# A gated-memory mixer and two MLPs on one core: the decay-and-rotation chain in fourteen steps instead of sixteen, with the pair of chunks ahead of the last one

## The reference

```python
def _attn_ref(q, k, v, a_re, a_im):                 # B, H, S, D = 4, 8, 768, 48
    mag = np.sqrt(a_re * a_re + a_im * a_im)
    scale = np.minimum(mag, 0.999) / (mag + 1e-06)
    a_re_n, a_im_n = (a_re * scale, a_im * scale)
    for t in range(S):
        ar, ai = (a_re_n[:, :, t, :, None], a_im_n[:, :, t, :, None])
        new_re = ar * S_re - ai * S_im
        new_im = ar * S_im + ai * S_re
        kv = np.einsum('bhd,bhe->bhde', k[:, :, t], v[:, :, t])
        S_re, S_im = (new_re + kv, new_im)
        y[:, :, t] = np.einsum('bhd,bhde->bhe', q[:, :, t], S_re)
def _moe_ref(x, w_in, w_out):                       # 3072 tokens, 384 -> 2048 -> 384
    h = x @ w_in
    g = h * np.clip(h + 3.0, 0.0, 6.0) / 6.0
    return g @ w_out
def _moe2_ref(x, w1, w2, w3, w_out):                # 384 -> 1024 twice, product, 1024 -> 1024 -> 384
    h = ((x @ w1) * (x @ w2)) @ w3
    return h @ w_out
```

## Time and profile before

| what | us |
|---|---|
| median of 3 runs (lowest, highest) | 1022.08 (1019.12, 1023.35) |
| the profiled execution's own time | 1022.37 |
| its span, first to last instruction | 1020.6 |
| busy: TensorE, VectorE, ScalarE, GpSimd | 910.4, 470.5, 430.5, 256.6 |
| first matmul of the first MLP | 101.53 |
| first MLP, units 0 to 7 | 101.53 to 712 |
| second MLP | 712 to 1020.6 |

### The profile page before, as it was taken

One profiled execution on the slowest core, in us unless ns is written; L12 is line 12 of the kernel. 1 busy time (PEld: TensorE's weight loads), 2 busy tenths in 40 slices (PEclk: granted clock), 3 DMA queues, 4 the chain that ended last, 5 costly groups with the idle time before them and its releaser, 6 DMA issues.

```text
span 1020.6 us, 14665 instructions
## 1 busy us (share of the span) xinstructions
PE 910.4 (89%) x5721; PEld 834.9 (82%) x5721; DVE 470.5 (46%) x610; ACT 430.5 (42%) x650; POOL 256.6 (25%) x200
## 2 busy tenths in 40 slices
PE   6944469889989989989989989989999999999996
PEld 3534468879889889889889889989888888888886
DVE  6445549849658648648748733233212121212110
ACT  4543535555655655555555532353212122212121
POOL 1011336222222222222222222343222222222221
PEclk9977769989989999999999999999999999999999
DMA  9584132353343343343344141510101010101000
GB/s 347 201 230 128 46 63 78 85 119 88 108 87 95 100 91 98 93 90 99 107 89 110 48 84 50 188 68 11 44 1 62 1 62 1 62 1 62 1 32 33
DMA packets 73688, 85.85 MB, mean 84 GB/s; under 512 B 6928, under 2 KB 59792, under 8 KB 73616
## 3 DMA queue, kind: packets, MB, share of 16 engines
q1 hardware_dynamic: 73216, 84.07, 29.7%
q10 hardware_dynamic: 400, 0.80, 0.5%
...
## 4 chain that ended last, share of the span: by engine, by line
issue 39%; PE 38%; POOL 14%; DVE 3%; ACT 2%; DMA 2%; SPq 1%; ACTq 0%; POOLq 0%; DVEq 0%
POOL gL L1328 13%; PE hb L937 10%; PE acc L959 7%; PE bQ L937 5%; PE bR L937 5%; PE bP L959 2%; PE hb L796 2%; PE acc L816 2%; PE acc L890 2%; DMA F<-QKs 1%; PE hb L890 1%; DVE QKc L1198 1%; DMA wo_sb<-in_moe_w_out_dram 1%; PE bQ L846 0%; PE bR L846 0%
## 5 line engine op out<-in xcount | busy, mean ns | idle before, releaser
L1328 POOL TENSOR_TENSOR gL<-g_sb,gH 128x384 fp32r<-128x384 f32 x128 | 157.1, 1227 | 428.2 <-ACT gH L1036 425.9
L796 PE MATMUL hb<-xHL,winH 128*128 128x384 f32 x768 | 168.6, 356 | 10.7 <-DMA xHL<-yHL 9.1
L816 PE MATMUL acc<-gH,woutH 128*128 128x384 f32 x384 | 134.0, 349 | 32.5 <-POOL gL L1328 23.6
L1237 DVE SCALAR_TENSOR_TENSOR g_sb<-t_sb,hb 128x384 f32<-128x384 f32 x128 | 70.4, 550 | 189.6 <-ACT t_sb L1046 105.8
L796 PEld LDWEIGHTS hb<-xHL,winH 128*128 128x128 f32 x768 | 140.2, 199 | 13.3 <-DMA xHL<-yHL 9.5
L1046 ACT ACTIVATE t_sb<-hb,cst 128x384 f32<-128x384 f32 x128 | 74.4, 581 | 154.1 <-PE hb L796 153.4
L816 PE MATMUL acc<-gH,woutL 128*128 128x384 f32 x384 | 133.3, 347 | 0.0
L816 PE MATMUL acc<-gL,woutH 128*128 128x384 f32 x384 | 132.8, 346 | 0.0
L1341 POOL TENSOR_TENSOR pL<-p_sb,pH 128x512 fp32r<-128x512 f32 x48 | 67.0, 1396 | 231.9 <-ACT pH L1098 231.9
L816 PEld LDWEIGHTS acc<-gH,woutH 128*128 128x128 f32 x384 | 75.0, 195 | 37.6 <-issue 29.3
L1036 ACT CAST gH<-g_sb 128x384 fp32r<-128x384 f32 x128 | 65.3, 510 | 79.4 <-DVE g_sb L1237 79.2
...
## 6 DMA issues: line engine op xcount, KB each, us to landing
...
```

Source lines behind the costliest of these rows:

```text
L796: mm = pe.matmul(o, w[:, kk * DF1 + ft * P:kk * DF1 + (ft + 1) * P], xv(u)[:, 2 * kk + part, :], start=(i == 0), stop=(i == 8))
L816: mm = pe.matmul(acc[m][:, 0:UNIT], w[:, ft * DM + m * P:ft * DM + (m + 1) * P], gg[:, (n % 3) * UNIT:(n % 3 + 1) * UNIT], start=(ft == 0 ...
L1237: dve.scalar_tensor_tensor(out=g_sb[:, :], in0=t_sb[:, :], scalar=6.0, in1=hb[n % 2][:, 0:UNIT], op0=ALU.min, op1=ALU.mult).then_inc(s["hs ...
L1328: pool.tensor_tensor(gL[:, (n % 3) * UNIT:(n % 3 + 1) * UNIT], g_sb[:, :], gH[:, (n % 3) * UNIT:(n % 3 + 1) * UNIT].bitcast(F32), ALU.subt ...
```

## The change

- The chain takes steps 0 to 13. ScalarE and VectorE's steps are dealt out anew: the arctangent moves from step 10 to 6, the sum of the angles from 11 to 7, the wrapped turns from 12 to 8 and 9, the exponentials of the magnitudes stand at 9, cos at 10, sin at 11.
- A fourth work tile, `W4`, holds the angles. For units 0 and 1 it lies over `gH` (`W4_early`), which the first MLP does not use yet; from unit 2 on it is `x2_sb`, the tile in which the first MLP's output is copied out. So there are new waits: the first three `gH` wait for unit 1's wrapped turns, `evac_x2_act` waits for the wrapped turns of a unit, and step 3 waits until `x2_sb` has been stored.
- The factor 1/pi was a ScalarE pass (L1020); it is now inside VectorE's instructions, which are one pass more.
- "Pairs first": the products with decays, cos and sin are done for chunks 0 and 1 at steps 10 and 12 and for chunk 2 at steps 11 and 13. The loads of q and k are split likewise: one DMA for the pair, one for the last chunk, in place of one for q and one for k.
- In a slot ScalarE does relu, `gH`, chunk work, chain step; VectorE does `g_sb`, chunk work, chain step.
- SyncE issues both halves of the pair scatter at step 13 and loads the next AR, AI at step 11; the store of the first MLP's output stands at slot 2, not 3.
- Units 0 and 1 of the chain, the splits of weights and the rows of `w3 @ w_out` stand at other slots; in unit 7 the second MLP's weights are split in halves over six slots.

```diff
+        W4_early = at("W4_early", KT * UNIT, F32, where[0] - 4 * (KT * UNIT + 6 * UNIT))
...
-        SPLIT_H = {(-1, 0): (0,), (-1, 8): (4,), (-1, 9): (1,), (0, 1): (5,), (0, 3): (2,), (0, 5): (6,), (0, 7): (3,), (0, 9): (7,)}
+        SPLIT_W = {(-2, 15): (0,), (-1, 3): (1,), (-1, 8): (4,), (0, 0): (2,), (0, 2): (5,), (0, 4): (3,), (0, 6): (6,), (0, 8): (7,)}
...
             if u == -1:
-                return ([(1, 0)] if sl == 0 else []) + ([(1, sl + 1)] if sl < 9 else [])
+                return [(1, sl)] if sl <= 10 else []
             if u == 0:
-                return {0: [(1, 10), (1, 11)], 1: [(1, 12), (1, 13)], 2: [(1, 14), (1, 15)],
-                        3: [(2, 0), (2, 1)], 15: [(2, 13), (2, 14), (2, 15)]}.get(sl, [(2, sl - 2)])
-            return [(u + 2, sl)] if u + 2 < NU else []
+                return {15: [(2, 12), (2, 13)]}.get(sl, [(2, sl - 3)] if sl >= 3 else [(1, sl + 11)])
+            return [(u + 2, sl)] if u + 2 < NU and sl < 14 else []
...
-        W3_COPY = {(-2, 9): (0, 1), (-2, 10): (2,), (-2, 11): (3, 4), (-1, 0): (5,), (-1, 1): (6,), (-1, 2): (7,)}
+        W3_COPY = {(-2, 8): (0, 1), (-2, 9): (2,), (-2, 10): (3, 4), (-2, 14): (5, 6), (-2, 15): (7,)}
...
@@ evac_x2_act @@
+            act.wait_ge(s["turns_wrapped"], min(u + 3, NU))
@@ SyncE @@
+            def load_pair(p):
...
+                    sp.wait_ge(s["f_pair_dma"], 16 * FD * p)
+                    sp.wait_ge(s["kT_psum"], 2 * (carried(CPU * p - 2) + 1))
+                sp.dma_start(qk(QKs)[:, 0:2 * KT, 0:2 * P], qk_src(p)[:, 0:2 * KT, :]).then_inc(s["pair_dma"], 16)
...
                     for p, t in steps(u, sl):
-                        if t == 12 and p + 1 < NU:
+                        if t == 11 and p + 1 < NU:
                             load_a(p + 1)
-                        if t == 14:
+                        if t == 13:
                             scatter_pair(sp, p, 0)
-                        if t == 15 and p > 0:
                             scatter_pair(sp, p, 1)
@@ ScalarE, pre @@
+                if t == 3:
+                    if p > 2:
+                        act.wait_ge(s["x2_stored"], 16 * KT * (p - 2))
+                    act.activation(W4(p)[:, :], W1[:, :], ACT.Exp, scale=-0.5).then_inc(s["exp_ln_mag"], 1)
...
+                if t == 6:
+                    act.wait_ge(s["atan_arg"], p + 1)
+                    act.activation(W2[:, :], W2[:, :], ACT.Arctan, scale=-1 / QUARTER_TURN).then_inc(s["atan_done"], 1)
-                if t == 12:
-                    act.wait_ge(s["turns_summed"], KT * (p + 1))
-                    act.mul(W2[:, :], W1[:, :], float(1 / np.pi)).then_inc(s["turns"], 1)
@@ ScalarE, the loop of slots @@
+                        high_g(n)
                         if sl == 1 and u > 0:
                             evac_x2_act(act, u - 1)
-                    if n is not None:
-                        for p, t in steps(u, sl):
-                            pre(p, t)
-                        high_g(n)
...
-                    if n is None:
-                        for p, t in steps(u, sl):
-                            pre(p, t)
+                    for p, t in steps(u, sl):
+                        pre(p, t)
...
-                    if u == NU - 1 and sl in (4, 6, 8):
+                    if u == NU - 1 and 3 <= sl < 9:
@@ VectorE, pre @@
+                if t == 12:
+                    dve.wait_ge(s["pair_decayed"], 2 * (p + 1))
                     dve.wait_ge(s["cos_turns"], p + 1)
                     for i in range(2):
-                        dve.tensor_tensor(part(QKc, i), part(QKs, i), tokens(W3), ALU.mult).then_inc(s["cos_rotated"], 1)
-                if t == 15:
+                        dve.tensor_tensor(pair(part(QKc, i)), pair(part(QKs, i)), pair(tokens(W2)), ALU.mult).then_inc(s["pair_cos"], 1)
                     dve.wait_ge(s["sin_turns"], p + 1)
                     for i in range(2):
-                        dve.tensor_tensor(part(QKs, i), part(QKs, i), tokens(W2), ALU.mult).then_inc(s["sin_rotated"], 1)
+                        dve.tensor_tensor(pair(part(QKs, i)), pair(part(QKs, i)), pair(tokens(W3)), ALU.mult).then_inc(s["pair_sin"], 1)
```

More of the change, by code:

```diff
@@ new lines, in pre, with pair @@
+                if t == 13:
+                    dve.wait_ge(s["last_decayed"], 2 * (p + 1))
+                    for i in range(2):
+                        dve.tensor_tensor(last(part(QKc, i)), last(part(QKs, i)), last(tokens(W2)), ALU.mult).then_inc(s["last_cos"], 1)
+                    for i in range(2):
+                        dve.tensor_tensor(last(part(QKs, i)), last(part(QKs, i)), last(tokens(W3)), ALU.mult).then_inc(s["last_sin"], 1)
+            def pair(v_):
+                return v_[:, :, 0:2, :]
@@ L1204, in part, with last @@
+            def last(v_):
+                return v_[:, :, 2, :]
             def part(t_, i):
```

208 lines of the change are left out of this document (103 added, 105 removed).

## The result

The changed kernel takes 983.95 us (median of 4 runs, 983.21 to 986.94) against 1022.27 before: a ratio of 0.9636, with a 95% interval of 0.9606 to 0.9665. The forecast was 974 with a range of 944 to 1004.

What follows compares the result with a forecast made beforehand. TensorE bounds the kernel (910.4 of 1020.6 us busy), losing time to waits and lower clock. Gains of 5.5 + 12 + 4 + 16 + 4 + 6.5 = 48 from 1022.4 give 974 us, range 944 to 1004.

Steps and rivals of the forecast that it cites:

- Start: Ahead of the first MLP: S gains 4.5 us, SyncE's stop at row stores goes; first matmul at 96.0, -5.5 us.
- Slots 0 to 4: Unit 0's first five slots: fewer chain steps there, so the scatter lands earlier; 33 against 44.9 us, -12.
- Rest of unit 0: Behind slot 4: clean length about 48 us, taken as 52 with four splits left, against 56.25; -4.
- Units 2 to 5: Waits for `gH`, `gL` and `F` go, some tiles come late; 71.5 us a unit.
- Unit 1: Two chain steps in the slot 15 ahead make `F` late: 4 us of wait and 1.5 of clock above 71.5.
- Units 6 and 7: Unit 6 loses its wait for `F`, 70.28 to 66.3 us; unit 7's halved splits shorten the `gL` hold, to 53.6.
- rival E: Chain's table loads: a change of tables costs twice what its load shows, units take 75.5 us; 994 us, chance 0.04.
- what comes: Units 1 to 5: more VectorE passes and fuller ScalarE slots make `Kc` and `g_sb` of tile 13 late; 5 to 6 us.
- Rival B: MLP units: tiles are not late, a unit is 67 us; 952 us in all, chance 0.2.
- Rival D: VectorE: steps behind chunk work and beside GpSimd's `gL` lengthen passes, a unit of 80.5 us; 1019 us, chance 0.06.
- Rival A: Scatter of `F` is still late, with waits and lower clock in six units; 996 us, chance 0.2.
- Rival C: Start and unit 0 give only half, since unit 1's steps 9 and 10 delay the first relu; 985 us, chance 0.15.

Runs made afterwards that it cites:

- table alone: Changed kernel with the old order inside a slot on both engines (chain step ahead of chunk work, on ScalarE also of `gH`): 958.4 us, 0.9375.
- order alone: Kernel before with only the new order inside a slot, its table of sixteen steps a unit kept: 1049.4 us, 1.0266.
- experiment 6: Changed kernel with the load of unit 1's AR and AI put behind the first pair scatter of `F`: 984.7 us, 0.9655.
- experiment 8: Changed kernel with GpSimd's subtractions for five weight pieces cut to 32 columns, low parts left out of the first MLP's result: 979.0 us, 0.9591.
- experiment 7: Changed kernel with unit 2's chain steps in unit 0 one slot earlier from slot 5, two in slot 4, one in slot 15: 986.4 us, 0.9664.
- experiment 4: Changed kernel with the splits of unit 7's weights whole again instead of six halves: 992.7 us, 0.9718.

## Why the prediction was right, and where it wasn't

| stretch | before | forecast | after | table alone | order alone |
|---|---|---|---|---|---|
| ahead of the first MLP | 101.5 | 96.0 | 99.8 | 101.5 | 103.7 |
| unit 0, slots 0 to 4 | 44.9 | 33 | 33.7 | 33.3 | 46.6 |
| rest of unit 0 | 56.3 | 52 | 56.2 | 53.1 | 55.2 |
| units 1 to 5 | 379.0 | 363 | 366.9 | 344.4 | 400.6 |
| unit 6 | 70.3 | 66.3 | 64.8 | 65.5 | 72.6 |
| unit 7 | 60.1 | 53.6 | 53.2 | 53.2 | 61.4 |

- **Start: -5.5 forecast, -1.7 measured.** S gained 0.7 (61.89 against 62.54 in the earlier trace rows) and not 4.5. The steps of VectorE came when foretold (sin products through at 47.0), but from the last scatter DMA's end of issue to S it took 7.5 us and not 4.8; experiment 6 shows that the load in front caused most of this (5.1 without it), and that it costs nothing in the end, since chunk 1 then waits for chunk 0's x store. The mis-sized terms are the landing time, and the thought that an earlier S brings an earlier first matmul.
- **Slots 0 to 4: -12 forecast, -11.2 measured**, all of it from the table, as argued. Slot 5 began at 133.5, not 129; 3.8 of that is the start.
- **Rest of unit 0: -4 forecast, -0.1 measured.** The failed step is "with four splits left in them I take 52". The splits cost VectorE 3.1 us at one pass and 1.9 at another, and the stretch 4.5 (experiment 8: 51.7 without them). The stretch ends with unit 1's first matmul, and so with a wait of 3.1 for x (3.0 before, 3.1 without the splits); with the old order that wait is 0.7, which is most of what the order costs here (53.1 against 56.2).
- **Units 2 to 5: 71.5 forecast, 71.3 measured.** The count of tiles was right in its places and its sum: `Kc` at slot 10 (0.9 of wait where 1.8 was forecast), `gemm1` of slot 15 (2.1 to 2.5, forecast 1.2 to 2.6), tile 10's lateness (1.0 at slot 12, forecast 2), no wait on `F`. (71.5 is 3.7 less than 75.2 and not 3.3; the forecast doesn't use that number.)
- **Unit 1: +5.5 forecast, +10.1 measured.** The wait for `F` was 0.8 and not 4: with two steps in slot 15, `g_sb` (1.8) and the copy-out of x (3.4) were late first; with one (experiment 7) these waits are 0 and 0.5, and the wait for `F` is 2.6.
- **Units 6 and 7: -4 and -6.5 forecast, -5.5 and -6.9 measured.** The halves carry unit 7 (experiment 4).
- **Second MLP, table loads**: 0.7 less where 0 was forecast. A table load is 1.28 and the next activation starts 1.3 behind its start (466.90 and 468.19), as the sum had it, and no unit from 2 on takes 75.5: rival E did not happen.

So the time came out by the forecast's own terms: the start (3.8), the rest of unit 0 (4.2) and units 1 to 5 (3.9) are 12 slower than forecast, and the other stretches give back 2, which leaves the miss of 10. The match of the sum is no luck, but it says nothing on what each half of the change is worth, and there the prediction was wrong. **What failed is a reason behind the sum: the order inside a slot was credited with a gain, and it costs 26 us.** The prediction said that the waits on `gH` and `gL` lose their cause since "`gH` is never behind a chain step". The table alone removes them but for one of 2.3 in unit 1: it spreads the knot of step 13, three passes and two table loads in one slot, over slots 10 and 11. The order alone removes them too, and puts longer waits for `g_sb` and the copy-out of x in their place. The late tiles that I counted under "what comes", 5 to 6 us a unit, I took as given with the change; 3.8 us a unit of them are the price of the new order (71.3 against 67.5). Rival B's "tiles are not late, a unit is 67" describes the table under the old order to 0.5 us. Rival D named the right danger, work that stands behind a wait for another engine, but put it on VectorE and in lengthened passes; it was ScalarE, and idle time. Rival A did not happen. Rival C (the start and unit 0 give only half) came true in part, 13 of 21.5, but not by a late first `g_sb`, which is 6.8 behind the first matmul and so inside its 8.

What stays open: whether `gH` alone, or the chunk copies too, make up the 20 to 27 us of ScalarE's order, and how the 64 us of the table divide beyond unit 7's halves.
